# Two heads side by side at lanes 0 to 95, one product for q and k, and token-down tiles spread over three slots

## The chip, the cores and the metric

One Trainium2 chip, of which the program uses one core. The metric is the device time of one execution in microseconds. A kernel's time is the median of its runs.

## The reference

Three layers stand one behind the other, in float32, for 4 batches of 768 tokens.

```python
# attention: q, k, v, alpha are (4, 8, 768, 48)
for t in range(S):
    state = alpha[:, :, t, :, None] * state + einsum('bhd,bhe->bhde', k[:, :, t], v[:, :, t])
    y[:, :, t] = einsum('bhd,bhde->bhe', q[:, :, t], state)
x = y, heads joined: (4, 768, 384)
# mixer
h = maximum(x.T @ w_tok1, 0) @ w_tok2        # over tokens, 768 -> 256 -> 768
u = x + h.T
x2 = u + maximum(u @ w_ch1, 0) @ w_ch2       # over channels, 384 -> 1536 -> 384
# channel mix: xk, xr mix x2 with the token before, weights mu_k, mu_r
out = sigmoid(xr @ w_r) * (maximum(xk @ w_k, 0) ** 2 @ w_v)
```

## The kernel before

**Attention.** A batch is cut into 6 chunks of 128 tokens and 4 pairs of heads: 24 steps. A step works on one pair in one chunk. TensorE transposes q, k and alpha of the pair, so that the head dimension lies along the lanes: head 0 at lanes 0 to 47, head 1 at lanes 64 to 111, with padding (0 for q and k, 1 for alpha) between them. VectorE makes running products of alpha, forwards (`decay`) and backwards (`suffix`), the reciprocal `rlast` of the last decay, and `qd` = q x decay, `kd` = k x suffix (L899 to L911). ScalarE spreads `qd` x `rlast` into a tile of 256 columns, with one head's lanes in the first 128 columns and the other's in the last (`spread_q`, L753); the rest of that tile is zero. TensorE makes the scores of both heads in one product, VectorE masks them into `am` (L928), TensorE computes y from `am`, v and the state (L540, L543) and the chunk's own k-v product from `kdt` (L546). VectorE adds that to the decayed state which GpSimd has made (`state_d`, L420), one instruction a head (L947).

**Precision.** Products in the mixer, and the scores of batches 1 to 3, are made as three products of high and low float32r parts. ScalarE writes the high part (L747, L758, L763, L767), VectorE the low one (L950, L918, L922, L975, L977).

**Mixer.** `token_up` gives two tiles (h1), `token_down` six tiles u (three for each half of the tokens), and 24 channel units follow, each with an up and a down product. The tiles use a ring of two PSUM banks. A token-down tile is six products of 384 columns (L599) and six of 256 columns that add x itself through a shifted identity (L605).

**Order.** Each engine has its own program, written out by hand in 28 slots. Batch 0 has attention alone (a pass of slots before the loop), while the mixer's weights are loaded and split in pieces: ScalarE makes the high part (L729) and GpSimd the low one (L413). Then a loop of three passes interleaves the attention of batch r with the mixer of batch r - 1. In slot s TensorE does the mixer's part, then y of step s - 2, the scores of step s - 1 and the transposes of step s. Slot 0 holds the second token_up tile (the first is made at the end of the pass before), slot 1 nothing of the mixer, slots 2 and 3 three token-down tiles each, and slots 4 to 27 the channel units. ScalarE and VectorE have the second h tile in slot 1, behind the attention of slot 0. The mixer of batch 3 runs alone after the loop, and then the channel mix for all batches.

GpSimd also adds up u (L429) in slots 8 to 13 of a pass. The small `omu` = 1 - mu (L1046) is made on VectorE between batch 0 and the loop.

Of the kernel before, what the change touches and what calls it, by code (L numbers as in the profile page):

```python
# [13 lines left out]
def attention_mixer_channel_mix(nc, q, k, v, alpha, w_tok1, w_tok2, w_ch1, w_ch2,  # L14
# [7 lines left out]
    P = 128  # L22
# [7 lines left out]
    DP = 64  # L30
# [22 lines left out]
    with ctx:  # L53
# [31 lines left out]
        def wr_w(n, kt):  # L85
# [11 lines left out]
        qka = [sb(f"qka{n}", [P, 3, H, DP]) for n in range(2)]  # L97
        vt = [sb(f"vt{n}", [P, NP, 2, W2]) for n in range(2)]
        decay = sb("decay", [P, 4, P])
        suffix = sb("suffix", [P, 2, P])  # L100
# [4 lines left out]
        kd = sb("kd", [P, 2, P])  # L105
# [18 lines left out]
        qka3 = [[buf[:, n, :, :] for n in range(3)] for buf in qka] + [  # L124
            [free_words[half][:, o:o + H * DP].rearrange("p (h d) -> p h d", h=H)
             for half, o in ((0, 0), (0, H * DP), (1, 0))]]
        qbd = free_words[1][:, H * DP:H * DP + 4 * P].rearrange("p (n t) -> p n t", n=2)
        vt3 = vt + [mixed[:, :, :].rearrange("p a t -> p (a t)")[:, 0:NP * 2 * W2]
                    .rearrange("p (a h e) -> p a h e", a=NP, h=2)]
        x2_in = [qka[n][:, :, :, :].rearrange("p a h d -> p (a h d)")[:, 0:KC * (HT + 1)]  # L130
                 .rearrange("p (c t) -> p c t", c=KC) for n in range(2)]
# [10 lines left out]
        def transposed_qka(r, i):  # L142

            b_tr = bank[5] if is_first(r) and i % 2 else bank[0]
            return b_tr[:, 0:P], b_tr[:, P:2 * P], b_tr[:, 2 * P:3 * P]

        def scores_kdT(r, i):

            b_sc = bank[7] if is_first(r) and i % 2 else bank[1]
            return b_sc[:, 0:2 * P], b_sc[:, 2 * P:3 * P]  # L150

        def y_kv(r, i):

            b_y = bank[6] if is_first(r) and i % 2 else bank[2]
            return b_y[:, 0:W2], b_y[:, P:P + W2]
# [18 lines left out]
        qd_ready = sem("qd_ready")  # L174
# [3 lines left out]
        kd_ready = sem("kd_ready")  # L178
# [94 lines left out]
        def _(sp):  # L273
# [95 lines left out]
            sp.wait_ge(consts_v, 14)  # L369
# [13 lines left out]
        def _(pool):  # L383
            def pad(n):

                for a, value in enumerate((0.0, 0.0, 1.0)):
                    nc.gpsimd.memset(qka3[n][a][:, :, D:DP], value).then_inc(consts_g, 1)

            pad(0)
            nc.gpsimd.memset(ident[:, :], 0.0).then_inc(consts_g, 1)  # L390
            pool.wait_ge(consts_g, 4)
            nc.gpsimd.affine_select(out=ident[:, :], in_=ident[:, :], compare_op=ALU.not_equal, fill=1.0,
                                    base=0, pattern=[[-1, P]], channel_multiplier=1).then_inc(consts_g, 1)
            nc.gpsimd.memset(causal[:, :], 1.0).then_inc(consts_g, 1)
            nc.gpsimd.memset(shift_f, 0.0).then_inc(consts_g, 1)
            pad(1)
            pad(2)
            pool.wait_ge(consts_g, 13)

            nc.gpsimd.affine_select(out=causal[:, :].rearrange("p (h t) -> p h t", h=2),  # L400
# [15 lines left out]
            def carry_state(r, i):  # L416
# [3 lines left out]
                nc.gpsimd.tensor_tensor(state_d[:, i % 4, :], state[:, i % NP, :],  # L420
                                        decay[:, i % 4, P - 1:P].to_broadcast([P, W2]), ALU.mult)\
# [57 lines left out]
        def _(pe):  # L479
# [7 lines left out]
            def transposes(r, i):  # L487
                c, p = step(i)
                qb, loads = chunk_buffer(r, c)
                if is_first(r) and i == 0:  # L490
                    pe.wait_ge(consts_g, 5)
                    pe.wait_ge(pair_loaded, 48)
                if is_first(r) and i == 1:
                    pe.wait_ge(consts_g, 15)
                if i % NP == (1 if is_first(r) and i < NP else 0):
                    pe.wait_ge(qka_loaded[qb], 48 * loads)
                if not isinstance(r, int):
                    pe.wait_ge(kd_ready, STEPS * r + i)
                elif i >= 2:
                    pe.wait_ge(kd_ready, i - 1)  # L500
                for n, dst in enumerate(transposed_qka(r, i)):
                    mm = nc.tensor.transpose(  # L502
                        dst, qka3[qb][n][:, 2 * p:2 * p + 2, :].rearrange("p h d -> p (h d)"), ident[:, :])
                mm.then_inc(tr_done, 1)

            def attention_scores(r, i):
                c, _ = step(i)
                pe.wait_ge(kd_ready, STEPS * r + i + 1)
# [6 lines left out]
                if c < NC - 1:  # L515
                    nc.tensor.transpose(kdT, kd[:, i % 2, :], ident[:, :])
                pe.wait_ge(qbd_ready, 2 * (STEPS * r + i + 1))
                if is_first(r):

                    mm = nc.tensor.matmul(scores, kd[:, i % 2, :], qbd[:, i % 2, :], start=True, stop=True)  # L520
                else:
                    pe.wait_ge(split_ready, 3 * (STEPS * (r - 1) + i + 1))
                    for n, (a, b) in enumerate(PASSES):
                        mm = nc.tensor.matmul(scores, ks[a][:, :], qs[b][:, :], start=(n == 0), stop=(n == 2))  # L524
# [598 lines left out]
```

## Time and profile before

| | |
|---|---|
| median of 3 runs | 802.19 us (802.06 to 802.52) |
| the profiled execution | 803.43 us, span 801.8 us |
| mean granted TensorE clock | 0.991 |
| TensorE busy | 776.8 us, 97% |
| VectorE busy | 483.1 us, 60% |
| ScalarE busy | 325.8 us, 41% |
| GpSimd busy | 96.9 us, 12% |
| batch 0's attention | about 5 to 59 us |
| the loop of three passes | about 59 to 468 us |
| mixer of batch 3 | about 468 to 577 us (the channel mix begins inside it) |
| channel mix | to 801.8 us |

A matmul's record begins where its columns start to stream and ends when the last result is out, so records of one engine overlap: the distance between two starts is what a matmul costs. The same holds for VectorE to a smaller degree. A row of the timeline gives the start and the length in us; "x3" means three records in one line, and the square bracket behind it is the engine's idle time before and who ended it.

### The profile page before, as it was taken

What the parts mean: (1) busy time and instruction counts of PE and PEld (TensorE: products, weight loads), DVE (VectorE), ACT (ScalarE), POOL (GpSimd) and SP (SyncE); (2) the same over time, 40 slices, a digit from 0 to 9 for tenths busy, and PEclk for the clock granted to TensorE, in tenths of its full rate; (3) what the DMA queues carried; (4) which work ended last, traced back from release to release, by engine and by line L of the source; (5) the groups of instructions that cost most, each with busy time, mean ns of one, the idle gap of its engine ahead of it and who ended that gap; (6) DMA issues with size and microseconds to landing.
All of it is one profiled execution on the core that took longest, in us unless ns stands there. A gap on an engine that the chain in (4) does not pass through costs nothing.

```text
span 801.8 us, 14717 instructions
## 1 busy us (share of the span) xinstructions
PE 776.8 (97%) x4864; PEld 764.0 (95%) x4864; DVE 483.1 (60%) x1467; ACT 325.8 (41%) x843; POOL 96.9 (12%) x142
## 2 busy tenths in 40 slices
PE   5998999999899999899999999999899999999998
PEld 4887999999899999899999999999899999999998
DVE  6987777872677776367777522243744744753751
ACT  4773433441343333144433313123643733743641
POOL 1665022100002110001210025001000000000000
PEclk9999999999999999999999999999999999999999
DMA  9974222332033232122222002301001101101000
GB/s 189 201 166 78 40 41 40 74 56 44 11 58 49 44 69 40 42 31 40 41 58 75 1 31 76 119 30 42 19 30 50 39 30 50 39 30 57 1 29 29
DMA packets 114895, 43.88 MB, mean 55 GB/s; under 512 B 102160, under 2 KB 112016, under 8 KB 114832
## 3 DMA queue, kind: packets, MB, share of 16 engines
q1 hardware_dynamic: 113680, 38.36, 22.8%
q0 software_dynamic: 1152, 4.72, 1.6%
q8 instruction: 35, 0.57, 0.3%
q14 instruction: 28, 0.23, 0.1%
HBM read 33.63 MB, written 9.44 MB: 54 GB/s over the span
## 4 chain that ended last, share of the span: by engine, by line
PE 85%; DVE 7%; issue 3%; ACT 2%; POOL 1%; DMA 1%; SPq 1%; DVEq 0%; ACTq 0%; POOLq 0%
PE bank L635 19%; PE bank L619 18%; PE bank L701 13%; PE bank L679 11%; PE bank L688 4%; PE bank L540 3%; PE bank L524 3%; PE bank L599 3%; PE bank L502 3%; PE bank L543 2%; PE bank L605 2%; PE bank L546 2%; PE bank L573 2%; DVE decay L899 1%; DMA qka<-in_alpha 1%
## 5 line engine op out<-in xcount | busy, mean ns | idle before, releaser
L758 ACT ACTIVATE qs_hi<-qd,rlast 64x128 fp32r<-64x128 f32 x144 | 57.6, 400 | 141.7 <-DVE qd L909 139.9
L975 DVE SCALAR_TENSOR_TENSOR hid_lo<-bank,hid_hi 128x384 fp32r<-128x384 f32 x96 | 53.1, 553 | 68.3 <-ACT hid_hi L767 68.3
L767 ACT ACTIVATE hid_hi<-bank 128x384 fp32r<-128x384 f32 x96 | 46.6, 485 | 68.9 <-PE bank L619 68.9
L846 ACT ACTIVATE relu_k<-bank 128x384 f32<-128x384 f32 x64 | 31.5, 492 | 102.8 <-PE bank L679 85.1
L619 PE MATMUL bank<-u_hi,wch_hi 128*128 128x384 f32 x288 | 71.1, 355 | 0.0
L918 DVE SCALAR_TENSOR_TENSOR qs_lo<-qd,rlast,qs_hi 64x128 fp32r<-64x128 f32 x144 | 52.3, 364 | 27.9 <-ACT qs_hi L758 25.6
L619 PE MATMUL bank<-u_lo,wch_hi 128*128 128x384 f32 x288 | 66.0, 337 | 0.0
L619 PE MATMUL bank<-u_hi,wch_lo 128*128 128x384 f32 x288 | 65.6, 335 | 0.0
L635 PE MATMUL bank<-hid_lo,wch_hi 128*128 128x384 f32 x288 | 65.5, 334 | 0.0
L635 PE MATMUL bank<-hid_hi,wch_hi 128*128 128x384 f32 x288 | 65.4, 334 | 0.0
L635 PE MATMUL bank<-hid_hi,wch_lo 128*128 128x384 f32 x288 | 65.4, 334 | 0.0
L1090 DVE TENSOR_TENSOR x_half<-bank,x_half 128x384 f32<-128x384 f32 x24 | 13.4, 558 | 77.5 <-PE bank L701 77.5
L502 PE MATMUL bank<-ident,qka 128*128 128x128 f32 x264 | 45.4, 283 | 9.2 <-POOL causal L400 4.1
L747 ACT ACTIVATE x_hi<-bank 128x96 fp32r<-128x96 f32 x96 | 23.9, 249 | 73.1 <-PE bank L546 56.7
L420 POOL TENSOR_TENSOR state_d<-state,decay 128x96 f32<-128x96 f32 x64 | 21.9, 346 | 258.8 <-DVE decay L899 258.8
L1073 DVE TENSOR_TENSOR relu_k<-relu_k 128x384 f32<-128x384 f32 x64 | 35.7, 558 | 27.9 <-ACT relu_k L846 26.4
L540 PE MATMUL bank<-vt,relu_k 128*128 128x96 f32 x352 | 51.4, 268 | 0.6 <-DVE relu_k L928 0.6
L619 PEld LDWEIGHTS bank<-u_lo,wch_hi 128*128 128x128 f32 x288 | 51.7, 188 | 0.0
L619 PEld LDWEIGHTS bank<-u_hi,wch_lo 128*128 128x128 f32 x288 | 51.6, 188 | 0.0
L540 PEld LDWEIGHTS bank<-vt,relu_k 128*128 128x128 f32 x352 | 50.0, 190 | 1.6 <-DVE relu_k L928 1.6
L635 PEld LDWEIGHTS bank<-hid_hi,wch_hi 128*128 128x128 f32 x288 | 51.2, 188 | 0.1
L635 PEld LDWEIGHTS bank<-hid_hi,wch_lo 128*128 128x128 f32 x288 | 51.3, 188 | 0.0
(124 smaller groups left out, 1837.1 us busy)
## 6 DMA issues: line engine op xcount, KB each, us to landing
w_raw<-in_moe_w_ch SPq DMA_DIRECT2D x12, 384.0 KB, 3.7
x_scratch<-x_half POOLq DMA_DIRECT2D x8, 576.0 KB, 3.5
out<-x_half SPq DMA_DIRECT2D x24, 192.0 KB, 1.9
vt<-in_v SPq DMA_DIRECT2D x44, 96.0 KB, 2.5
qka<-in_q SPq DMA_DIRECT2D x21, 192.0 KB, 3.1
qka<-in_k SPq DMA_DIRECT2D x21, 192.0 KB, 3.9
qka<-in_alpha SPq DMA_DIRECT2D x21, 192.0 KB, 4.1
qka<-x_scratch SPq DMA_DIRECT2D x4, 577.5 KB, 3.9
```

The costliest lines, as they stand in the source:

```text
L502: mm = nc.tensor.transpose(dst, qka3[qb][n][:, 2 * p:2 * p + 2, :].rearrange("p h d -> p (h d)"), ident[:, :])
L540: mm = nc.tensor.matmul(y_ps, am[:, i % 2, h * P:(h + 1) * P], vt3[vb][:, p, h, :], start=(h == 0), stop=(h == 1 and c == 0))
L619: mm = nc.tensor.matmul(dst, ch1_w(a, n % KC, jj), u[c][:, n % KC, half * HT:(half + 1) * HT], start=(n == 0), stop=(n == 3 * KC - 1))
L635: mm = nc.tensor.matmul(b_acc[m][:, 0:HT], ch2_w(a, jj, m), hid[c][:, j % HJ, :], start=(jj == 0 and n == 0), stop=(jj == NJ - 1 and n == 2))
L679: mm = nc.tensor.matmul(dst, wk_w(a, n % KC, j), mix_out[0][c][:, n % KC, :], start=(n == 0), stop=(n == 3 * KC - 1))
L688: mm = nc.tensor.matmul(b_acc[m][:, 0:DM], mix_out[1][a][:, n % KC, m * P:(m + 1) * P], wr_w(c, n % KC), start=(n == 0), stop=(n == 3 * KC ...
L701: mm = nc.tensor.matmul(bank[m][:, 0:DM], k2[a][:, n % NF, m * P:(m + 1) * P], wv_w(c, n % NF), start=(n == 0), stop=(n == 3 * NF - 1))
L758: nc.scalar.activation(dst[lanes, h * P:(h + 1) * P], qd[lanes, i % 4, :], ACT.Copy, scale=rlast[lanes, i % 4:i % 4 + 1])\
L767: nc.scalar.activation(dst, b_ring[t % 2][:, 0:HT], func).then_inc(tile_hi, 1)
L918: nc.vector.scalar_tensor_tensor(qs[1][lanes, cols], qd[lanes, i % 4, :], rlast[lanes, i % 4:i % 4 + 1], qs[0][lanes, cols], ALU.mult, ALU ...
L975: ins = nc.vector.scalar_tensor_tensor(dst, src, 0.0, hi, ALU.max, ALU.subtract)
L1073: nc.vector.tensor_tensor(relu_k[:, j % 2, :], relu_k[:, j % 2, :], relu_k[:, j % 2, :], ALU.mult).then_inc(k2_ready, 1)
```

## The change

- The heads of a pair lie unpadded at lanes 0 to 47 and 48 to 95. All per-step tiles use lanes 0 to 95. The padding fills on GpSimd go, and with them TensorE's wait for them.
- Where the code used to pick a head's lanes by their number, it now multiplies by a mask column: `head` (128 x 2) has ones at a head's lanes. A new VectorE instruction makes `rhead` = head x rlast, one column a head. ScalarE's spread and VectorE's low part take it as their scalar over all 96 lanes, and the state update becomes (k-v product x head) + state_d in one instruction.
- `decay` and `suffix` lie side by side, so do q and k in PSUM, and one product of 256 columns makes `qkd`, which holds qd and kd. ScalarE's spread waits for this product.
- `rhead` has to wait for the reciprocal in front of it.
- The token-down tiles are two a slot in slots 1 to 3. In a tile the products with the second h tile come last, behind the residual products. ScalarE and VectorE make the second h tile in slot 0, after that slot's attention.
- Four zero fills before the loop go.

```diff
-        qd = sb("qd", [P, 4, P])
+        rhead = sb("rhead", [P, 4, 2])
+        head = sb("head", [P, 2])
+        qkd = sb("qkd", [P, 4, 2, P])
...
-                if is_first(r) and i == 1:
-                    pe.wait_ge(consts_g, 15)
...
-                    nc.tensor.transpose(kdT, kd[:, i % 2, :], ident[:, :])
+                    nc.tensor.transpose(kdT, kd[0:W2, i % 4, :], ident[0:W2, 0:W2])
...
-                    mm = nc.tensor.matmul(kv_ps, kdt[:, i % 2, :],
+                    mm = nc.tensor.matmul(kv_ps, kdt[:, i % 2, 0:W2],
...
             def token_down(b, half, m):
...
+                for kt in range(KT):
+                    for n, (i, j) in enumerate(PASSES):
...
+                        mm = nc.tensor.matmul(dst, h1[i][:, kt, m * P:(m + 1) * P], tok2_w(j, kt, half),
+                                              start=(kt == 0 and n == 0), stop=(kt == KT - 1 and n == 2))
+                    if kt > 0:
+                        continue
+                    for n in range(TM):
...
 (mixer_part, TensorE)
-                elif s < FIRST_UNIT:
-                    pe.wait_ge(w_lo_ready, TOK2_END)
-                    for m in range(KC):
-                        token_down(b, s - KT, m)
+                elif s < FIRST_UNIT:
+                    if s == 1:
+                        pe.wait_ge(w_lo_ready, TOK2_END)
+                    for n in (2 * s - 2, 2 * s - 1):
+                        token_down(b, *divmod(n, KC))
...
 (spread_q, ScalarE)
-                act.wait_ge(qd_ready, STEPS * r + i + 1)
+                act.wait_ge(qkd_ready, STEPS * r + i + 1)
                 for h in range(2):
-                    lanes = slice(h * DP, (h + 1) * DP)
-                    nc.scalar.activation(dst[lanes, h * P:(h + 1) * P], qd[lanes, i % 4, :], ACT.Copy,
-                                         scale=rlast[lanes, i % 4:i % 4 + 1])\
+                    nc.scalar.activation(dst[0:W2, h * P:(h + 1) * P], qd[0:W2, i % 4, :], ACT.Copy,
+                                         scale=rhead[0:W2, i % 4, h:h + 1])\
...
 (loop pass, ScalarE; VectorE has second_low in the same place)
                     mixer_part(r - 1, s)
                     attention_part(r, s)
+                    if s == 0:
+                        second_high(r - 1)
...
 (scale_qk, VectorE)
-                nc.vector.tensor_tensor(qd[:, i % 4, :], qT, decay[:, i % 4, :], ALU.mult).then_inc(qd_ready, 1)
+                dve.wait_ge(rlast_ready, G + 1)
+                nc.vector.tensor_scalar(rhead[0:W2, i % 4, :], head[0:W2, :], rlast[0:W2, i % 4:i % 4 + 1], None,
+                                        ALU.mult).then_inc(rhead_ready, 1)
                 dve.wait_ge(suffix_ready, G + 1)
-                nc.vector.tensor_tensor(kd[:, i % 2, :], kT, suffix[:, i % 2, :], ALU.mult).then_inc(kd_ready, 1)
+                nc.vector.tensor_tensor(qkd[0:W2, i % 4, :, :],
+                                        transposed_qka(r, i)[:, 0:2 * P].rearrange("p (n t) -> p n t", n=2),
+                                        decays[0:W2, i % 4, :, :], ALU.mult).then_inc(qkd_ready, 1)
...
 (outputs, VectorE)
-                            ins = nc.vector.tensor_tensor(own, kv, state_d[lanes, i % 4, h * D:(h + 1) * D], ALU.add)
+                            ins = nc.vector.scalar_tensor_tensor(own, kv_ps[:, cols], head[0:W2, h:h + 1],
+                                                                 state_d[0:W2, i % 4, cols], ALU.mult, ALU.add)
```

## Rows read from the trace of the kernel before

**Rows 1.** The page's part 1: busy us, share of the span, instructions.

```profile
PE 776.8 (97%) x4864; PEld 764.0 (95%) x4864; DVE 483.1 (60%) x1467; ACT 325.8 (41%) x843; POOL 96.9 (12%) x142
```

**Rows 2.** Windows: us, busy us and instructions of each engine, granted clock, DMA.

```profile
20.00:40.00 20.00, 19.81 (x145) 17.49 (x144) 19.55 (x91) 15.48 (x45) 12.12 (x15) 1.00 1.08 200
...
197.00:223.00 26.00, 23.59 (x149) 22.18 (x147) 15.95 (x53) 9.27 (x26) 0.81 (x1) 0.93 0.19 45
```

**Rows 3.** Timeline, batch 0, VectorE: start us, length us, instruction.

```profile
24.04 0.14 DVE L908 RECIPROCAL rlast<-decay 128x1 f32<-128x1 f32 x1
24.09 0.27 DVE L909 TENSOR_TENSOR qd<-bank,decay 128x128 f32<-128x128 f32 x1
...
24.48 0.41 DVE L947 TENSOR_TENSOR state<-bank,state_d 64x48 f32<-64x48 f32 x2
...
24.92 0.26 DVE L950 TENSOR_TENSOR x_lo<-bank,x_hi 128x96 fp32r<-128x96 f32 x1
...
26.07 0.14 DVE L908 RECIPROCAL rlast<-decay 128x1 f32<-128x1 f32 x1
```

**Rows 4.** Timeline, the second step's transposes.

```profile
7.64 0.87 PE L502 MATMUL bank<-ident,qka 128*128 128x128 f32 x3 [2.66 <-DMA qka<-in_alpha]
```

**Rows 5.** Timeline, head of the second loop pass.

```profile
199.27 1.20 PE L573 MATMUL bank<-x_hi,wtok_lo 128*128 128x384 f32 x6
...
200.78 0.82 ACT L758 ACTIVATE qs_hi<-qd,rlast 64x128 fp32r<-64x128 f32 x2 [5.75 <-DVE qd L909]
...
201.64 0.73 DVE L918 SCALAR_TENSOR_TENSOR qs_lo<-qd,rlast,qs_hi 64x128 fp32r<-64x128 f32 x2 [0.69 <-ACT qs_hi L758]
...
202.60 0.55 DVE L975 SCALAR_TENSOR_TENSOR h_lo<-bank,h_hi 128x384 fp32r<-128x384 f32 x1
...
202.74 0.39 PE L524 MATMUL bank<-qs_hi,ks_hi 128*128 128x256 f32 x1 [1.42 <-DVE ks_lo L922]
...
218.81 0.77 PE L619 MATMUL bank<-u_hi,wch_hi 128*128 128x384 f32 x3
```

**Rows 6.** Timeline, batch 0, ScalarE and GpSimd.

```profile
22.36 0.82 ACT L758 ACTIVATE x_half<-qd,rlast 64x128 f32<-64x128 f32 x2 [0.44 <-DVE qd L909]
...
24.11 0.24 ACT L747 ACTIVATE x_hi<-bank 128x96 fp32r<-128x96 f32 x1
24.13 1.81 POOL L413 TENSOR_TENSOR wtok_lo<-w_raw,wtok_hi 128x768 fp32r<-128x768 f32 x1 [1.65 <-ACT wtok_hi L729]
...
25.91 0.65 POOL L420 TENSOR_TENSOR state_d<-state,decay 128x96 f32<-128x96 f32 x2
```

**Rows 7.** Timeline, between batch 0 and the first loop pass.

```profile
59.15 3.64 POOL L413 TENSOR_TENSOR wch_lo<-w_raw,wch_hi 128x768 fp32r<-128x768 f32 x2 [0.39 <-ACT wch_hi L729]
59.29 1.73 DVE L1046 TENSOR_SCALAR omu<-mu 128x6 f32<-128x6 f32 x1
```

**Rows 8.** Timeline, first token-down tiles of batch 3.

```profile
471.40 0.33 PE L599 MATMUL bank<-wtok_hi,h_hi 128*128 128x384 f32 x1
...
473.71 0.34 PE L599 MATMUL bank<-wtok_hi,h_hi 128*128 128x384 f32 x1
...
475.47 0.44 PE L599 MATMUL bank<-wtok_hi,h_hi 128*128 128x384 f32 x1
```

**Rows 9.** Timeline, slot 4 of the second loop pass.

```profile
220.85 0.69 PE L540 MATMUL bank<-vt,relu_k 128*128 128x96 f32 x4 [0.20 <-DVE relu_k L928]
```

**Rows 10.** Timeline, a steady slot of the first loop pass.

```profile
127.96 0.29 DVE L922 TENSOR_TENSOR ks_lo<-kd,ks_hi 128x128 fp32r<-128x128 f32 x1
...
128.72 0.39 PE L546 MATMUL bank<-vt,relu_k 128*128 128x96 f32 x2
...
128.94 0.27 PE L516 MATMUL bank<-ident,kd 128*128 128x128 f32 x1
...
129.41 0.49 PE L502 MATMUL bank<-ident,qka 128*128 128x128 f32 x3
...
129.66 0.60 PE L619 MATMUL bank<-u_hi,wch_hi 128*128 128x384 f32 x2
```

More of the change, by code:

```diff
@@ L523, in attention_scores @@
                     for n, (a, b) in enumerate(PASSES):
-                        mm = nc.tensor.matmul(scores, ks[a][:, :], qs[b][:, :], start=(n == 0), stop=(n == 2))
+                        mm = nc.tensor.matmul(scores, ks[a][0:W2, :], qs[b][0:W2, :], start=(n == 0), stop=(n == 2))
                 mm.then_inc(scores_done, 1)
@@ L767, in tile_high, with second_high @@
                 nc.scalar.activation(dst, b_ring[t % 2][:, 0:HT], func).then_inc(tile_hi, 1)
+            def second_high(b):
+                tile_high(b, 1, h1[0][:, 1, :], ACT.Relu)
             def mixer_part(b, s):
-                if s < KT:
-                    tile_high(b, s, h1[0][:, s, :], ACT.Relu)
+                if s == 0:
+                    tile_high(b, 0, h1[0][:, 0, :], ACT.Relu)
                 elif s < FIRST_UNIT:
-                    half = s - KT
-                    if half == 0:
+                    if s == 1:
                         act.wait_ge(x2_base, 2 * KC * b + 1)
-                    for m in range(KC):
-                        tile_high(b, KT + KC * half + m, u[0][:, m, half * HT:(half + 1) * HT], ACT.Copy)
+                    for n in (2 * s - 2, 2 * s - 1):
+                        half, m = divmod(n, KC)
+                        tile_high(b, KT + n, u[0][:, m, half * HT:(half + 1) * HT], ACT.Copy)
                 else:
@@ L940, in outputs @@
                     for h in range(2):
-                        lanes = slice(h * DP, (h + 1) * DP)
-                        kv = kv_ps[lanes, h * D:(h + 1) * D]
-                        own = state[lanes, p, h * D:(h + 1) * D]
+                        cols = slice(h * D, (h + 1) * D)
+                        own = state[0:W2, p, cols]
                         if c == 0:
-                            ins = nc.vector.tensor_copy(own, kv)
+                            ins = nc.vector.tensor_scalar(own, kv_ps[:, cols], head[0:W2, h:h + 1], None, ALU.mult)
                         else:
-                            ins = nc.vector.tensor_tensor(own, kv, state_d[lanes, i % 4, h * D:(h + 1) * D], ALU.add)
+                            ins = nc.vector.scalar_tensor_tensor(own, kv_ps[:, cols], head[0:W2, h:h + 1],
+                                                                 state_d[0:W2, i % 4, cols], ALU.mult, ALU.add)
                     ins.then_inc(state_ready, 1)
@@ L1040, in _ @@
                     last_constants()
-            for n in range(2):
-                for h in range(2):
-                    nc.vector.tensor_copy(qs[n][:, h * P:(h + 1) * P], zeros[:, :]).then_inc(consts_v, 1)
-            dve.wait_ge(consts_v, 13)
             dve.wait_ge(mu_loaded, 32)
```

160 lines of the change are left out of this document (81 added, 79 removed).

## The prediction

> **What bounds the kernel now.** I read the page first. TensorE is busy 97% of the span [rows 1]. That number alone says little, since matmuls overlap, so I cut the span into stretches [rows 2] and asked in each which engine never rests. Three kinds of stretch come out.
>
> From 16 to 58 us, the attention of batch 0, VectorE is busy 19.55 of 20 us [rows 2]. The timeline shows it as a chain without a hole: reciprocal follows reciprocal after 2.03 us [rows 3], the same from 16 us to 54.5 us, 19 times. This stretch costs what a VectorE step costs. Before 16 us the loads set the pace: the second transposes wait until 7.64 us for alpha [rows 4].
>
> Inside the three loop passes TensorE has no gaps (steady slots of 4.8 us) except at the head. There the stretch 197 to 223 us shows 23.59 us of work in 26 and a mean granted clock of 0.93 [rows 2]; the head of each pass looks alike. A mean of 0.93 means that twice the missing 0.07, 0.14 x 26 = 3.6 us, ran at 1.2 GHz instead of 2.4, in which half the work is lost, so it costs 1.8 us. It comes directly after TensorE stood waiting.
>
> The last part (mixer of batch 3, feed forward) is TensorE work that the change leaves alone, but for one place.
>
> **The change, part by part.** (a) *The VectorE step in batch 0.* Removed: qd and kd, which together take 24.48 - 24.09 = 0.39 us from start to start [rows 3]. Added: one product of 256 columns. An instruction of 128 columns takes 0.27 us [rows 3], one of 384 takes 0.55 [rows 5]; 256 lie at 0.41, and start to start about 0.08 less as qd shows, so 0.33. Added too: the head-masked scalar rhead, which waits for the reciprocal's own end. The reciprocal takes 0.14 and its successor now starts after 0.05 [rows 3]; with the wait it is 0.14 plus the length of a signal. Between engines that is 0.04 (ScalarE's spread ends at 200.78 + 0.82, qs_lo starts at 201.64 [rows 5]). That makes 0.18, plus rhead's own start to start, 0.05 to 0.12. So recip to state goes from 0.44 to 0.18 + 0.09 + 0.33 = 0.60, that is +0.16. The two state updates and the start of x_lo now take 24.92 - 24.48 = 0.44 [rows 3]; their durations (0.41 for two) leave no overlap, as between different lanes. With all at lane 0 I take the usual overlap: two times 0.18 = 0.36, so -0.08. They now read a per-lane scalar; qs_lo, which does, takes 0.365 against qd's 0.27, so up to +0.1 each. Bounds of the step: 0 and +0.35. I take +0.08.
>
> Two waits follow. ScalarE's x_hi ends at 24.35 and state starts at 24.48 [rows 3, 6]: it has about 0.1 us to spare. ScalarE's spread starts at 22.36 [rows 6], 0.35 us after its reciprocal (one step before the one at 24.04, so at 22.01), and must wait for the whole product, 0.18 + 0.09 + 0.41 + 0.04 = 0.72 after it. So spread, the weight split behind it and x_hi (in the order of ScalarE) slip by 0.37, while state slips by 0.16 + 0.08: a stall of about 0.1 in each step with a weight piece, every second one. And rhead has its only company on GpSimd: state_d behind the long split (25.91 for 0.65 [rows 6]) meets the rhead of the second step; say 0.1 to 0.15 again. Per pair of steps 0.16 + 0.1 + 0.13 = 0.39; some 9 pairs bound by VectorE, so +3.5. Taken off: the four zero fills before the passes, which VectorE doesn't need now, 0.3. **+3.2**, bounds 0 and +8.
>
> A row speaks against rhead. The small omu, 128x6, took 1.73 us and ended as the first of two GpSimd splits ended (59.15 to 60.97) [rows 7]. It is the one other tensor_scalar from SBUF to SBUF, as rhead is. The splits take 1.81 us and start at 24.13, 0.09 after the reciprocal [rows 6]. In the new order the split starts 0.36 later for the spread and rhead 0.18 after its reciprocal, which itself is 0.08 to 0.16 later: rhead is ahead of the split by 0.1 to 0.2 us. I take it that it gets through. The Trainium skill, "SBUF — State Buffer", section Who interferes with whom, says that a tensor_scalar in a two-port mode and a GpSimd instruction lock one shared port pair, and whoever comes first blocks the other for its whole length. The omu row agrees; by that rule the cost hangs on the order of two starts, and is my third rival.
>
> (b) *Loop heads.* Now in slot 0, TensorE ends token_up (a row of six 384-column matmuls lasts 1.20 [rows 5], the last of them 0.34 [rows 8], so one starts every 0.86 / 5 = 0.173; 199.27 + 6 x 0.173 = 200.31), then waits for kd and for ks_lo until 202.74 [rows 5]; only 0.3 us of work lies between. It then runs 3.6 us at half clock. Two slots carry three tiles and slot 1 none; the first channel tile starts at 218.81 [rows 5]. New: at 200.31 tile 0 of token-down can start (its h tile is long done). A tile is 1.76 us [rows 8]; three hi/lo products of 384 columns (0.52) and six residual products (1.76 - 6 x 0.173 = 0.72) go by before it needs the second h tile, at 201.55. ScalarE makes that behind the spread: the spread started at 200.78, now 0.37 later (201.15 to 201.97), ks_hi about 0.2, then 0.49: 202.68. TensorE idles 1.15, does 0.35, and waits for h_lo: VectorE is then at ks_lo, with h_lo behind it (202.60 for 0.55 now [rows 5]) about 0.2 later, until 203.35. It ends the tile at 203.5, the second at 205.3. Slot 1's scores and transposes are 129.66 - 128.72 less kdt's 0.22 = 0.72 [rows 10]; slots 2 and 3 add kdt and four passes of 0.11 for y, 1.38, and two tiles, 4.9 each: 215.8 against 218.81 if the clock stays at 2.4 GHz. Gain 3.0, or 1.2 if it falls as now. The waiting adds up to 1.5 us against 2.1 before; I take it that the clock holds. In pass 1 GpSimd is still splitting weights and rhead and qs_lo wait for it (omu again [rows 7]), and h_lo stands behind them on VectorE and TensorE behind h_lo: gain between 0 and 2, taken 0.9. Sum for three passes **-6.9**, bounds -9 and -2.
>
> Slot 4 has one channel tile only as cover (1.56 us), and TensorE already waits for the mask there (0.20 and a gap before it [rows 9]). The mask comes 0.16 later: **+0.5** for three passes. In steady slots the cover is twice as long: ks_lo ends at 128.25, TensorE comes to the scores behind kd's transpose of 128.94 [rows 10], 0.7 later, and 0.3 of that goes. If that cover were gone, 0.3 x 66 slots = 20 us would be lost; nothing here takes 0.7 away, and it is outside the range like rival three.
>
> (c) *Narrower operands on TensorE.* kdt has 96 weight columns rather than 128: its two passes start at 128.72, the next instruction at 128.94 [rows 10]: 0.22, 0.11 each. The three transposes have 96 weight columns too and still 128 moving: 129.66 - 129.41 = 0.25, 0.083 each. The trace has no narrower weight load. Nothing is the lower bound (moving columns set it), a quarter of both the upper: 0.055 + 0.062 = 0.12 us a step, and 0.01 for kd's transpose. Over 72 steps in gapless passes that is 0 to 9 us. 96 moving columns at 2.4 GHz would be 0.04, so the 0.11 is not their streaming in one pass; I take a third of the bound, 0.04 a step: **-3.0**. The Trainium skill, "TensorE: Matmul & The Clock Gate", section LDWEIGHTS, has the load go with the number of columns, columns / 1.2 ns: 107 ns for 128 and 80 for 96. The 0.11 a pass agrees, the transposes' 0.083 doesn't. By the page, as an estimate, kdt and transposes would give 5 x 0.027 = 0.13 a step, all of my upper bound, and the sum would be 6 us lower.
>
> (d) *Mixer of batch 3.* Its first token-down tile takes 473.71 - 471.40 = 2.31 us against 1.76 for the next [rows 8]; it waits for the second h tile. The residual products now stand in that wait: **-0.55**.
>
> (e) *Nothing:* the fills of the pads and the wait for them (the DMA of [rows 4] comes later); masks, 96 instead of 128 lanes on ScalarE, VectorE and GpSimd, since an instruction's time goes by its columns (two copies of 64 lanes x 48 columns take 0.41 [rows 3], one of 128 x 128 takes 0.27); DMAs, which move the same rows. The state updates in the passes become unlocked too, off the path.
>
> **Sum.** +3.2 - 6.9 + 0.5 - 3.0 - 0.55 = -6.8 us. The profiled execution had a span of 801.8 and a time of 803.43; the median of the runs is 802.19, 1.24 lower. From the median: 802.19 - 6.8, rounded to 795.
>
> **The rivals.** *Two: the gain at the heads is eaten.* TensorE still waits 1.5 us per head; if that lets the clock fall, passes 2 and 3 give 1.2 each and pass 1 nothing: 2.4. With the batch 0 step at +0.2 (+5) and no gain from narrow weights: 802.19 + 5 - 2.4 + 0.5 - 0.55 = 804.7; with (a) as taken and 1.5 from (c), 801.4. For it: the clock falls in all three heads now. Against: the wait is shorter and broken by work. I put it at 802.
>
> *Three, slower: rhead falls behind the weight split.* Place: the batch 0 steps with a piece. If rhead's start is later than the split's start, VectorE stands for what is left of 1.81 us. Some 10 pieces there x 1.7 = 17: 795 + 17 = 812. It decides at 0.1 to 0.2 us: one more signal delay of that size on VectorE does it. For it: omu. Against: the order that I worked out.
>
> *Four: narrow operands pay in full.* (c) at -8.5 and (a) at +1.5: 802.19 + 1.5 - 6.9 + 0.5 - 8.5 - 0.55 = 788. For it: both TensorE blocks are slower than their moving columns. The rule of the Trainium skill named in (c) leads here.
>
> **How the numbers follow.** Forecast 0.48, rival two 0.21, three 0.15, four 0.16. The range reaches from rival four's far side, 787, to 803 above rival two, and leaves out three and slivers. The forecast's own range is 790 to 799. 0.2% is 1.6 us, about what a measurement can tell. Faster by more: forecast and four, and half of two, less a little: 0.73. Within: 0.10. Slower: rival three and the end of two: 0.17.
>
> **What would show it.** Batch 0: reciprocals 2.2 us apart instead of 2.03, rhead about 0.18 after the reciprocal with a length near 0.1 (1.8 if rival three). Heads: one TensorE wait of about 1.2 us inside the first token-down tile and one of 0.3; granted clock 1.0 in all 26 us (0.93 if rival two); from first transposes to first channel tile 19 us instead of 22. Steady slots of 4.75 instead of 4.79 us; kdt passes below 0.11. Wrong would be: state updates with a mask much dearer than copies, rhead held up, a wait for ks_lo in the steady slots.

## The result, and the profile after

The kernel is 1.3% slower: 812.6 us (median of 4 runs, 811.34 to 812.82) against 802.2 (802.06 to 802.52), ratio 1.0126, 95% interval 1.0108 to 1.0143. The forecast was 795.0 with a range of 787 to 803; what came is its third rival, priced at 812 and given 0.15. The profiled execution has a span of 810.8 us against 801.8, so the spans differ by 9.0.

To see where they lie I took, on TensorE, the first transposes of each pass and the first token_up product of batch 3's mixer. Before, pass 1 begins at 59.32 us and batch 3's mixer at 468.28; after, at 78.25 and 477.94. So batch 0 grew by 18.93 us, the three passes shrank by 9.27 (408.96 to 399.69), and the rest shrank by 0.66. The heads of passes 2 and 3 are as forecast, that of pass 1 gains more; batch 0 lost almost twice what all the rest gained.

Windows of the kernel after: two in batch 0, and the head of pass 2, which begins at 212.27 here, for the 197 to 223 of [rows 2] (us, busy us and instructions of PE, PEld, DVE, ACT, POOL, granted clock, DMA):

```profile
20.00:40.00 20.00, 14.85 (x95) 12.49 (x95) 19.79 (x61) 9.04 (x30) 8.96 (x11) 0.91 0.67 142
40.00:64.00 24.00, 21.38 (x122) 18.45 (x123) 23.51 (x76) 12.12 (x39) 9.55 (x12) 0.79 0.59 147
212.00:238.00 26.00, 24.34 (x162) 23.13 (x163) 18.20 (x62) 9.05 (x30) 1.15 (x2) 1.00 0.19 48
```

VectorE is as full as before (19.79 of 20), but with 61 instructions where [rows 2] had 91: they have become long, or one has. The head of pass 2 has the granted clock at 1.00 instead of 0.93.

Timeline of VectorE in batch 0 after, for [rows 3] (start us, length us, instruction):

```profile
23.05 0.13 DVE L909 RECIPROCAL rlast<-decays 96x1 f32<-96x1 f32 x1
23.22 0.22 DVE L914 TENSOR_SCALAR rhead<-head,rlast 96x2 f32<-96x2 f32 x1
23.35 0.41 DVE L917 TENSOR_TENSOR qkd<-bank,decays 96x256 f32<-96x256 f32 x1
23.69 0.43 DVE L955 SCALAR_TENSOR_TENSOR state<-bank,head,state_d 96x48 f32<-96x48 f32 x2
24.04 0.24 DVE L959 TENSOR_TENSOR x_lo<-bank,x_hi 128x96 fp32r<-128x96 f32 x1
...
25.18 0.13 DVE L909 RECIPROCAL rlast<-decays 96x1 f32<-96x1 f32 x1
25.35 1.79 DVE L914 TENSOR_SCALAR rhead<-head,rlast 96x2 f32<-96x2 f32 x1
27.05 0.41 DVE L917 TENSOR_TENSOR qkd<-bank,decays 96x256 f32<-96x256 f32 x1
...
28.87 0.13 DVE L909 RECIPROCAL rlast<-decays 96x1 f32<-96x1 f32 x1
```

The same rhead of two elements a lane takes 0.22 us in one step and 1.79 in the next. A free step is 25.18 - 23.05 = 2.13 us long, the held one 28.87 - 25.18 = 3.69. Of the last 20 of batch 0's 24 steps ten are held (1.78 to 1.80 us, one 1.42), of the first four none. ScalarE and GpSimd in the same stretch, for [rows 6]:

```profile
23.80 0.69 ACT L754 ACTIVATE x_half<-qkd,rhead 96x128 f32<-96x128 f32 x2 [0.88 <-DVE qkd L917]
24.40 0.83 ACT L726 ACTIVATE wtok_hi<-w_raw 128x768 fp32r<-128x768 f32 x1
```

```profile
25.31 1.80 POOL L411 TENSOR_TENSOR wtok_lo<-w_raw,wtok_hi 128x768 fp32r<-128x768 f32 x1 [2.07 <-ACT wtok_hi L726]
```

GpSimd's split starts at 25.31, rhead at 25.35, and rhead ends as the split ends. In nine of the ten held steps the split is ahead by 0.03 or 0.04 us; in the one of 1.42 it is ahead by 0.41, and there too rhead ends as the split ends. In the passes a GpSimd instruction of 1.01 us (the residual preparation) holds rhead in six slots of each:

```profile
121.99 0.35 POOL L418 TENSOR_TENSOR state_d<-state,decays 96x96 f32<-96x96 f32 x1 [4.39 <-DVE decays L900]
...
122.23 1.10 DVE L914 TENSOR_SCALAR rhead<-head,rlast 96x2 f32<-96x2 f32 x1
...
122.30 1.01 POOL L427 TENSOR_TENSOR x_half<-u_hi,u_lo 128x384 f32<-128x384 f32 x1
```

Here rhead starts 0.07 us ahead of the long instruction and is held all the same: it starts 0.24 inside state_d's product, and GpSimd goes on to the long one without a gap. In the slots where state_d's product (0.34) stands alone, rhead takes 0.22 or 0.23. So a start ahead of the long instruction need not be enough when GpSimd is already at work. The slots with the residual preparation last 4.86 us where their neighbours last 4.75.

Head of pass 2 after, for [rows 5] (TensorE, with the idle time ahead of an instruction and who ended it in brackets):

```profile
212.27 0.53 PE L498 MATMUL bank<-ident,qka 128*96 128x128 f32 x3 [0.60 <-issue]
218.05 0.44 PE L595 MATMUL bank<-wtok_hi,h_hi 128*128 128x384 f32 x1 [0.88 <-ACT h_hi L762]
...
231.36 0.78 PE L616 MATMUL bank<-u_hi,wch_hi 128*128 128x384 f32 x3
```

From the first transposes to the first channel tile it is 231.36 - 212.27 = 19.09 us; before it was 218.81 - 196.80 = 22.01, the transposes there being these:

```profile
196.80 0.54 PE L502 MATMUL bank<-ident,qka 128*128 128x128 f32 x3 [0.73 <-issue]
```

In the steady slots kdt's pair goes by faster, for [rows 10]:

```profile
110.67 0.33 PE L542 MATMUL bank<-vt,relu_k 128*96 128x96 f32 x2
110.84 0.25 PE L512 MATMUL bank<-ident,qkd 96*128 96x96 f32 x1
...
111.31 0.49 PE L498 MATMUL bank<-ident,qka 128*96 128x128 f32 x3
```

0.17 us for the pair against 0.22. Batch 3, for [rows 8]: the first token-down tile lasts 482.81 - 481.06 = 1.75 us instead of 2.31.

```profile
481.06 0.33 PE L595 MATMUL bank<-wtok_hi,h_hi 128*128 128x384 f32 x1
...
482.81 0.33 PE L595 MATMUL bank<-wtok_hi,h_hi 128*128 128x384 f32 x1
```

### The profile page after: what moved, and what is told of

Same layout as the page of the kernel before. It is cut to its first block, busy times and chain, and to the rows that moved or that the text cites. A ratio compares the mean times of both kernels' runs of the same rounds, so it can differ in the third digit from the quotient of the medians.

```text
span 810.8 us, 14704 instructions
## 1 busy us (share of the span) xinstructions
PE 780.6 (96%) x4864; PEld 764.8 (94%) x4864; DVE 509.8 (63%) x1462; ACT 303.5 (37%) x843; POOL 96.1 (12%) x136
## 4 chain that ended last, share of the span: by engine, by line
PE 87%; DVE 6%; issue 3%; ACT 2%; SPq 1%; DMA 1%; DVEq 0%; ACTq 0%
PE bank L632 19%; PE bank L616 18%; PE bank L698 13%; PE bank L676 11%; PE bank L536 4%; PE bank L685 4%; PE bank L520 4%; PE bank L498 3%; PE bank L595 3%; PE bank L539 2%; PE bank L602 2%; PE bank L569 2%; PE bank L542 1%; PE bank L516 1%; DVE decays L900 1%
## 5 line engine op out<-in xcount | busy, mean ns | idle before, releaser
L754 ACT ACTIVATE qs_hi<-qkd,rhead 96x128 fp32r<-96x128 f32 x144 | 50.1, 395 | 172.6 <-DVE qkd L917 172.6
L927 DVE SCALAR_TENSOR_TENSOR qs_lo<-qkd,rhead,qs_hi 96x128 fp32r<-96x128 f32 x144 | 45.9, 358 | 30.5 <-ACT qs_hi L754 30.5
L914 DVE TENSOR_SCALAR rhead<-head,rlast 96x2 f32<-96x2 f32 x96 | 53.2, 555 | 3.5
L536 PEld LDWEIGHTS bank<-vt,relu_k 128*128 128x128 f32 x352 | 51.9, 196 | 2.1 <-DVE relu_k L937 2.0
L418 POOL TENSOR_TENSOR state_d<-state,decays 96x96 f32<-96x96 f32 x64 | 22.0, 344 | 257.8 <-DVE decays L900 257.8
L498 PE MATMUL bank<-ident,qka 128*96 128x128 f32 x264 | 45.6, 283 | 7.1 <-DMA qka<-in_alpha 6.0
L632 PEld LDWEIGHTS bank<-hid_lo,wch_hi 128*128 128x128 f32 x288 | 51.3, 188 | 0.0
```

Of the source, the lines that this page charges most:

```text
L498: mm = nc.tensor.transpose(transposed_qka(r, i)[:, n * P:(n + 1) * P], qka3[qb][n][:, 2 * p:2 * p + 2, :].rearrange("p h d -> p (h d)"), i ...
L536: mm = nc.tensor.matmul(y_ps, am[:, i % 2, h * P:(h + 1) * P], vt3[vb][:, p, h, :], start=(h == 0), stop=(h == 1 and c == 0))
L632: mm = nc.tensor.matmul(b_acc[m][:, 0:HT], ch2_w(a, jj, m), hid[c][:, j % HJ, :], start=(jj == 0 and n == 0), stop=(jj == NJ - 1 and n == 2))
L754: nc.scalar.activation(dst[0:W2, h * P:(h + 1) * P], qd[0:W2, i % 4, :], ACT.Copy, scale=rhead[0:W2, i % 4, h:h + 1])\
L914: nc.vector.tensor_scalar(rhead[0:W2, i % 4, :], head[0:W2, :], rlast[0:W2, i % 4:i % 4 + 1], None, ALU.mult).then_inc(rhead_ready, 1)
L927: nc.vector.scalar_tensor_tensor(qs[1][0:W2, cols], qd[0:W2, i % 4, :], rhead[0:W2, i % 4, h:h + 1], qs[0][0:W2, cols], ALU.mult, ALU.subt ...
```

## The experiments

Three theories were open for batch 0. A: rhead waits for GpSimd, and the order of two starts decides. B: VectorE's added work and its dependent wait fill batch 0, held or not. C: TensorE's lower granted clock in batch 0 (0.79 to 0.91) lengthens its steps. For the part that gained, the question was whether the tiles did it or the rest of the change. Diffs are against the changed kernel unless said otherwise.

**rhead read from two tiles.** The mask is 0 or 1, so the result is the same number.

```diff
-                nc.vector.tensor_scalar(rhead[0:W2, i % 4, :], head[0:W2, :], rlast[0:W2, i % 4:i % 4 + 1], None,
-                                        ALU.mult).then_inc(rhead_ready, 1)
+                nc.vector.scalar_tensor_tensor(rhead[0:W2, i % 4, :], head[0:W2, :], rlast[0:W2, i % 4:i % 4 + 1],
+                                               head[0:W2, :], ALU.mult, ALU.mult).then_inc(rhead_ready, 1)
```

> rhead is made by an instruction of VectorE in the same place and with the same waits, but it reads two tiles (mask column times 1/d times the mask again, which is 0 or 1), where the changed kernel's reads one tile and a column of scalars. Theory A, the ten long rheads: in the changed kernel rhead takes 0.22 us alone and 1.79 us where GpSimd's split of a weight has started before it, and if only the one-tile form waits for GpSimd, rhead is short in all 20 steps here. Ten times 1.57 us come back, and some 2 us more in the passes, where 18 rheads beside the residual preparation take 1.10 us: 794 to 796 us, transposes of pass 1 begin near 62. Theory B, VectorE's own work (one more instruction a step and the dependent wait ahead of it) fills batch 0: that is unchanged here, 812. Theory C, the lower granted clock of TensorE in batch 0 (0.79 to 0.91) makes the steps long: the clock and the time stay, 812. If the two-tile form is held up as well, the time stays at 812 with rheads of 1.8 us, and the run says nothing against A.

Measured: 813.03 us, ratio to before 1.0122 (1.0105 to 1.0139), the same as the changed kernel. This form is held as well, with the split at 25.33:

```profile
25.37 1.78 DVE L914 SCALAR_TENSOR_TENSOR rhead<-head,rlast 96x2 f32<-96x2 f32 x1
```

So my guess that only the one-tile form waits was wrong, and the run decides nothing between A and B. It does speak against C: the granted clock in 20 to 40 us was 0.74 here against 0.91 in the changed kernel, and the steps are as long (2.12 free and 3.70 held, one of 4.06). The Trainium skill, "SBUF — State Buffer", section Who interferes with whom, lists an instruction of VectorE with two SBUF inputs among those that contend with GpSimd; this row agrees (1.78 us), and had I read that line closely the run would have been spared.

**rhead made by ScalarE.**

```diff
 (scale_qk, VectorE)
-                if is_first(r) and i == 0:
-                    dve.wait_ge(consts_g, 7)
-                dve.wait_ge(rlast_ready, G + 1)
-                nc.vector.tensor_scalar(rhead[0:W2, i % 4, :], head[0:W2, :], rlast[0:W2, i % 4:i % 4 + 1], None,
-                                        ALU.mult).then_inc(rhead_ready, 1)
...
 (spread_q, ScalarE)
+                act.wait_ge(rlast_ready, STEPS * r + i + 1)
+                nc.scalar.activation(rhead[0:W2, i % 4, :], head[0:W2, :], ACT.Copy,
+                                     scale=rlast[0:W2, i % 4:i % 4 + 1]).then_inc(rhead_ready, 1)
+                act.wait_ge(rhead_ready, STEPS * r + i + 1)
                 act.wait_ge(qkd_ready, STEPS * r + i + 1)
```

> rhead is made by ScalarE, ahead of its wait for the two products, and VectorE does not make it at all. Theory A: no instruction of VectorE meets GpSimd's split any more, and VectorE is rid of the instruction and of its wait (0.13 + 0.22 us a step): a step of batch 0 of 1.9 to 2.0 us instead of 2.13 alone and 3.69 beside a split, 788 to 793 us. Theory B says 1.9 to 2.0 us a step as well, so this run alone does not tell A from B; it does together with the two-tile one. Theory C: 812. Against all: ScalarE now has one more instruction ahead of the spread, and if it is the engine that sets the step in the passes, the 60 steps grow by up to 0.2 us, 800 us or above.

Measured: 788.5 us, ratio 0.9822 (0.9805 to 0.9838). Steps of batch 0 are 1.94 us in the mean, and pass 1 begins at 57.23. The instruction takes 0.29 us on ScalarE, inside a split too (27.36, in the split of 27.26 to 29.08):

```profile
27.26 1.82 POOL L411 TENSOR_TENSOR wtok_lo<-w_raw,wtok_hi 128x768 fp32r<-128x768 f32 x1 [1.46 <-ACT wtok_hi L726]
...
27.36 0.29 ACT L754 ACTIVATE rhead<-head,rlast 96x2 f32<-96x2 f32 x1
```

As A and B said alike. The rival about ScalarE in the passes falls: the slots are 4.75 us, with the residual preparation too.

**The split 0.2 us later.** One small copy to a spare tile stands ahead of each rounding of a weight piece in batch 0; rhead is untouched.

```diff
 (batch 0, ScalarE)
                 attention_part(0, s)
                 for n in pieces_in(s):
+                    nc.scalar.activation(spare[:, n % 32, :], head[:, :], ACT.Copy)
                     split_hi(n)
```

> Nothing is changed in rhead; ScalarE has one small copy to a spare tile (0.2 us) ahead of each rounding of a weight piece in batch 0, so that GpSimd's split of the piece starts some 0.2 us later. It leaves the computation as it is. Theory A with the order of the two starts deciding (in the changed kernel the split starts 0.03 to 0.04 us ahead of rhead in the ten long cases): rhead is ahead now and short, 795 to 799 us. Theory A without the order (rhead waits whenever a split runs at any time of it): rhead overlaps the split's start and takes most of 1.8 us again, 812. Theories B and C: 812, or a little more for the added copy.

Measured: 796.63 us, ratio 0.993 (0.9914 to 0.9947), 16.0 us below the changed kernel, though ScalarE has an instruction more for each piece. VectorE and GpSimd:

```profile
24.28 0.22 DVE L916 TENSOR_SCALAR rhead<-head,rlast 96x2 f32<-96x2 f32 x1
...
26.41 0.41 DVE L916 TENSOR_SCALAR rhead<-head,rlast 96x2 f32<-96x2 f32 x1
```

```profile
24.34 1.85 POOL L412 TENSOR_TENSOR wtok_lo<-w_raw,wtok_hi 128x768 fp32r<-128x768 f32 x1 [1.98 <-ACT wtok_hi L727]
26.14 0.65 POOL L419 TENSOR_TENSOR state_d<-state,decays 96x96 f32<-96x96 f32 x2
```

rhead now starts 0.06 us ahead of the split and takes 0.22; starting 0.04 behind it, it took 1.79. That is the order of the starts, and theory B, whose work is all still here, falls: the steps are 2.13 us, and 2.32 in the six where state_d's two products, one behind the other (0.65), hold the next rhead for 0.2. One rhead (at 44.17) also starts inside a product of state_d, 0.06 us ahead of a split that follows without a gap, as in the passes, and yet takes 0.22; no run shows what sets it apart. The 18 holds in the passes are left (1.09 us, slots of 4.86).

**The tiles alone, on the kernel before.** Only token_down's new order, two tiles a slot in slots 1 to 3, and the second h tile behind slot 0's attention; the heads stay padded and q and k apart.

```diff
-                if s < KT:
-                    if s == 0:
-                        token_up(b, 1)
+                if s == 0:
+                    token_up(b, 1)
                 elif s < FIRST_UNIT:
-                    pe.wait_ge(w_lo_ready, TOK2_END)
-                    for m in range(KC):
-                        token_down(b, s - KT, m)
+                    if s == 1:
+                        pe.wait_ge(w_lo_ready, TOK2_END)
+                    for n in (2 * s - 2, 2 * s - 1):
+                        token_down(b, *divmod(n, KC))
```

> The kernel before with the rearranged token-down tiles alone: heads padded to lanes 0 and 64 as they were, no merged product, no rhead. My reading of the two traces: the loop heads give 2.9 to 4.0 us each, less 0.5 for slot 4, 8.0 to 8.7 us in the three passes, and 0.6 in batch 3: 793 to 794.5 us, with batch 0 as before (transposes of pass 1 near 59.3). Rival: the shorter heads of the changed kernel came from the rest of the change (the queue of VectorE is shorter), and the tiles alone give under 3 us: 799 to 802.

Measured: 793.17 us, ratio 0.9878 (0.9861 to 0.9894): 9.1 us off, so the rival falls. In the profiled executions (793.9 against 801.8) the passes last 401.8 us against 408.96 and batch 0 is as before (59.17). So the tiles alone carry 7.2 of the 9.27 us by which the changed kernel's passes shrank, and the 0.6 in batch 3.

**rhead as two instructions of one column.**

```diff
+                for h in range(2):
+                    ins = nc.vector.tensor_scalar(rhead[0:W2, i % 4, h:h + 1], head[0:W2, h:h + 1],
+                                                  rlast[0:W2, i % 4:i % 4 + 1], None, ALU.mult)
+                ins.then_inc(rhead_ready, 1)
```

> rhead is made in the same place by two instructions of one column each (96x1) where the changed kernel has one of two columns (96x2). The two-input form was held up as long as the one-input form (1.78 us), so what the instruction reads beside the mask is not what counts; every other instruction of VectorE in batch 0 reads a bank, or has a single element a lane: the reciprocal (96x1, from SBUF) takes 0.13 us even inside GpSimd's work. Theory D, one element a lane is not held up: two short instructions in all 20 steps, the 10 waits of 1.57 us gone, 0.1 us a step more for the second instruction, 795 to 798 us. Theory E, whatever reads and writes SBUF alone waits for GpSimd, and the reciprocals were only ahead of the split: 812, perhaps with the wait at the reciprocal in other steps.

Measured: 796.8 us, ratio 0.9935 (0.9913 to 0.9958). The pair takes 0.33 us though it starts 0.04 behind the split, as the held ones of the changed kernel do:

```profile
24.53 0.33 DVE L915 TENSOR_SCALAR rhead<-head,rlast 96x1 f32<-96x1 f32 x2
```

```profile
24.49 1.81 POOL L411 TENSOR_TENSOR wtok_lo<-w_raw,wtok_hi 128x768 fp32r<-128x768 f32 x1 [2.05 <-ACT wtok_hi L726]
```

Theory D holds, E falls: engine, form, place and data are the same, and what differs is one element a lane instead of two. The changed kernel has a row that agrees: a reciprocal (96x1, SBUF alone) that started 0.24 us inside a split (at 58.35) took 0.13. Each step pays 0.11 us for the second instruction (2.24), and in the passes the slots with the residual preparation take 4.75 as their neighbours do. Pass 1 begins at 65.09, 4.5 us later than in the next kernel. The steps are 2.5 of it: the last product of q and k starts at 58.34 against 55.86. The other 2.0 lie behind it, where the granted clock was 0.50 (1.2 GHz) in 60 to 65 us; why it fell there and not in the next kernel was not tried.

**The mask read from a bank.** It is copied once into two free columns of the transposes' banks.

```diff
+                head_ps = (bank[5] if is_first(r) and i % 2 else bank[0])[:, 3 * P:3 * P + 2]
+                if is_first(r) and i < 2:
+                    nc.vector.tensor_copy(head_ps, head[:, :]).then_inc(head_copied, 1)
+                    dve.wait_ge(head_copied, i + 1)
-                nc.vector.tensor_scalar(rhead[0:W2, i % 4, :], head[0:W2, :], rlast[0:W2, i % 4:i % 4 + 1], None,
+                nc.vector.tensor_scalar(rhead[0:W2, i % 4, :], head_ps[0:W2, :], rlast[0:W2, i % 4:i % 4 + 1], None,
                                         ALU.mult).then_inc(rhead_ready, 1)
```

> rhead is the same one instruction of two columns in the same place, but it reads the mask from two free columns of the bank that its step's transposes lie in (copied there once) and not from SBUF. Theory F, an instruction of VectorE that reads a bank is never held up by GpSimd, as the products, the mask copies and the state steps of batch 0 show: rhead 0.22 us in all steps, 794 to 797 us. Theory G, the size or form of the instruction alone is what holds it: ten rheads of 1.8 us again, 812.

Measured: 792.31 us, ratio 0.9888 (0.986 to 0.9916), 20.3 us below the changed kernel and 1.7 below the range expected for F. Again 0.04 us behind a split, and free:

```profile
28.06 1.82 POOL L412 TENSOR_TENSOR wtok_lo<-w_raw,wtok_hi 128x768 fp32r<-128x768 f32 x1 [1.82 <-ACT wtok_hi L727]
```

```profile
28.10 0.21 DVE L919 TENSOR_SCALAR rhead<-bank,rlast 96x2 f32<-96x2 f32 x1
```

Pass 1 begins at 60.59, so without the hold batch 0 costs 1.27 us more than before: steps of 2.12 and none held. F holds. That leaves 18.93 - 1.27 = 17.7 us, in two parts. Up to the last product of q and k (71.50 in the changed kernel, 55.86 here) it is 15.6, of which the ten holds are 15.3 (nine of 1.57 and the short one of 1.2). The other 2.0 come behind it, up to pass 1 (6.75 us against 4.73, for the same work): there TensorE, which had waited 2.38 us for the last spread, ran at half clock. The changed kernel first, then this one:

```profile
72.00:78.25 6.25, 5.47 (x21) 5.07 (x21) 1.72 (x7) 3.47 (x8) 2.48 (x2) 0.50 0.40 128
```

```profile
57.00:60.59 3.59, 3.37 (x20) 2.85 (x21) 1.30 (x5) 2.35 (x6) 2.48 (x3) 1.00 0.41 110
```

The windows of the steps settle theory C:

```profile
20.00:40.00 20.00, 18.71 (x140) 16.11 (x138) 19.68 (x86) 12.91 (x43) 11.69 (x15) 1.00 0.89 192
40.00:64.00 24.00, 21.72 (x148) 19.26 (x149) 19.59 (x82) 15.21 (x45) 15.71 (x12) 1.00 0.60 160
```

The clock is at 1.00 here, where TensorE need not stand through the holds. In the changed kernel it was at 0.91 and 0.79, but VectorE, with hardly a gap in 20 to 40 us, set the steps, and a free step has the same 2.12 or 2.13 us at either clock. So in the steps the clock followed and cost nothing; what it cost is the 2.0 us behind them.

**kdt with 128 stationary columns again.**

```diff
-                    mm = nc.tensor.matmul(kv_ps, kdt[:, i % 2, 0:W2],
+                    mm = nc.tensor.matmul(kv_wide(r, i), kdt[:, i % 2, :],
```

> The changed kernel with the two kdt products of a step back at 128 stationary columns (96 now); nothing else. My reading: a pair takes 0.17 us in the changed kernel and took 0.22 in the one before, TensorE is full in the passes, so 0.05 us in each of 60 steps are lost again: 3 us, 815 to 816. Rival: the gain of the steady slots (4.80 to 4.75 us) came from elsewhere (the state steps and the spread of VectorE and ScalarE being shorter): no change, 812.

Measured: 815.15 us, ratio 1.016 (1.0134 to 1.0185), 2.6 us above the changed kernel. The runs of the two spread over 811.3 to 812.8 and 813.0 to 815.5; the profile says it more surely:

```profile
111.44 0.39 PE L546 MATMUL bank<-vt,relu_k 128*128 128x96 f32 x2
111.67 0.25 PE L516 MATMUL bank<-ident,qkd 96*128 96x96 f32 x1
```

0.23 us for the pair against 0.17, and free slots of 4.81 against 4.75. Slots with a held rhead hardly grow (4.87): there VectorE sets the slot, and a faster TensorE buys nothing. (A zero fill before batch 0 grows with this edit too.)

**ScalarE's rhead, and the second h tile ahead of the spread.** Diff against the kernel of 788.5 us; VectorE makes the tile's low half ahead of split_low in the same way.

```diff
 (loop pass, ScalarE)
                     mixer_part(r - 1, s)
-                    attention_part(r, s)
                     if s == 0:
                         second_high(r - 1)
+                    attention_part(r, s)
```

> rhead on ScalarE, as in the kernel of 788.5 us, and in slot 0 ScalarE makes the second h tile ahead of the spread of its step, VectorE its low half ahead of the low halves of q and k. In the changed kernel TensorE waits 0.88 and 0.3 us in the first token-down tile of each pass for that h tile. If the tile's lateness sets the head: 2 to 3.5 us less, 785 to 786.5. Rival: the spread is later by the tile's 0.6 us, and the scores of the next slot wait as long: 788 to 789, the wait only moved.

Measured: 783.65 us, ratio 0.9769 (0.9747 to 0.9791): 4.9 us below that kernel, 18.5 below the one before, the fastest here, and a little below the 785 to 786.5 that I expected. Pass 1 (from its first transposes to those of pass 2) goes from 135.15 to 131.47 us, pass 2 from 132.18 to 130.59. The large share is pass 1's. With the tile late, TensorE waited there, and its clock was at 0.70 in 64 to 69 us:

```profile
64.87 0.45 PE L595 MATMUL bank<-wtok_hi,h_lo 128*128 128x384 f32 x1 [2.45 <-DVE h_lo L985]
```

With the tile early that wait is gone, the clock is 1.00 in 57 to 66 us, and the longest wait there is this one, for the scores, which the tiles now cover:

```profile
64.69 0.38 PE L520 MATMUL bank<-qs_hi,ks_hi 96*128 96x256 f32 x1 [0.19 <-DVE ks_lo L932]
```

## Why the prediction was wrong, step by step

**The step that failed** stands in (a): "rhead is ahead of the split by 0.1 to 0.2 us. I take it that it gets through". It is behind by 0.04. Its own start was right (0.17 us after the reciprocal, forecast 0.18), and so was the spread's (0.75 after it, forecast 0.72). What I left out is that the spread itself gets shorter, which (e) had put at nothing: its two instructions of 64 lanes started at lanes 0 and 64 and took 0.82 us; with 96 lanes each, both starting at lane 0, they overlap to 0.69, and the rounding behind them starts 0.60 after the spread instead of 0.85. Before, on ScalarE, beside the spread at 22.36 of [rows 6]:

```profile
23.21 0.84 ACT L729 ACTIVATE wtok_hi<-w_raw 128x768 fp32r<-128x768 f32 x1
```

From the spread's start to the split's it was 24.13 - 22.36 = 1.77 and is 25.31 - 23.80 = 1.51. These 0.26 us turn a lead of 0.1 to 0.2 into the measured lag. I had used just this overlap for VectorE's two state steps and not for ScalarE. The readings show the shorter time; that it is the lanes that make it was not tried by itself.

Behind it stands a second fault, of judgement. The margin was a tenth of a microsecond, made of several estimated terms, each uncertain by about as much, and the price of losing it was 17 us. I gave it 0.15 and left it outside the range. A term with that ratio of price to margin is a toss, and the range had to reach it. The price was right in size: 17 forecast for ten holds, 15.6 measured up to the last of them, and 2.0 more at half clock behind them, which the forecast had not. That rival three's 812 came within 1 us is partly luck: its terms were too high by 1.4 us for the holds, 1.9 for batch 0 without them, 0.5 for slot 4 and 2.4 for the head of pass 1, and it lacked the 2.0 of half clock and 2.0 of holds in the passes, which I had not thought of. The residual preparation costs there 6 slots x 0.11 x 3 = 2.0 us, shown by the slots of 4.75 instead of 4.86 in each kernel whose rhead isn't held.

**(a) without the hold:** +3.2 forecast, +1.3 measured (the mask from a bank). The step grew by 0.09 us (0.08 forecast), 2.12 or 2.13 for 2.03, and the stalls I had added for x_hi and state_d are not there. Where rhead reads SBUF and is ahead of the split (the later split), state_d's is there, 0.2 us in six steps for the 0.1 to 0.15 forecast, and batch 0 costs +2.7 (pass 1 begins at 62.00). The masked state steps cost hardly more than the plain ones (0.43 for two against 0.41).

**(b) heads:** -6.9 + 0.5 forecast. The tiles alone shortened the three passes by 7.2. In pass 2, 2.92 was measured for 3.0, by the steps named: a wait inside the first tile (0.88 for 1.15), a second of about 0.3, and a clock that holds at 1.00. Rival two falls. The +0.5 for slot 4 did not come: from its first channel tile to the next slot's it was 222.94 - 218.81 = 4.13 us and is 235.47 - 231.36 = 4.11.

In pass 1, 3.3 was measured (from 23.24 to 19.9) against 0.9 forecast, and 1.9 of it go with the late start of the pass. In the four kernels whose pass 1 begins by 62.0 us with the h tile in its place behind the spread (ScalarE's rhead, the later split, the tiles alone, the mask from a bank) the same stretch lasts 21.8 to 22.0 us, a gain of 1.2 to 1.5; in the four that come there at 65.1 us or later (the changed kernel, the two tiles, the single columns, the wide kdt) it lasts 19.7 to 20.3. TensorE's wait for h_lo is a little shorter in the changed kernel (2.06 us, against 2.46 with the mask from a bank), and its granted clock stays at 1.00 (84 to 90 us), against 0.72 (66 to 72 us) there. So part of what the late start of pass 1 cost came back at its head; why the clock held was not tried.

**(c) narrower operands:** -3.0 forecast; kdt is worth 2.6 in the runs and 0.055 us a free slot, so the size is right, but its make-up is not: I had spread it over kdt and transposes. All of it is kdt, 0.085 a pass instead of 0.11. The three transposes with 96 weight columns still take 0.25 (93.00 to 93.25). The Trainium skill's rule in "TensorE: Matmul & The Clock Gate", section LDWEIGHTS, fits kdt (107 to 80 ns by the page, 110 to 85 here) and not the transposes, so rival four falls.

**(d) batch 3:** -0.55 forecast, -0.56 measured. **(e)** held but for the spread on ScalarE, above.

**The sum.** The passes gave 9.27 against 9.4 forecast, though with 2.0 lost in them that I hadn't seen and 2.4 won in pass 1. The case that the forecast of 795.0 describes, rhead from SBUF and ahead of the split, is the kernel with the later split: 796.6. With no hold anywhere (the mask from a bank) it is 792.3, but 1.6 us of its gain in the profiled execution lie behind batch 3's first tile, in work that the change leaves alone; the granted clock was 1.00 in its channel mix (560 to 700 us) and 0.99 before (568 to 708 us).

What stays open: by what means the bank's and the single column's rhead escape (the runs show only that they do), why rhead is held when it starts just ahead of a long instruction but inside a short one (in the 18 slots of the passes, though not at 44.17 of the later split), why the spread's two instructions overlap more, and why the clock fell behind batch 0 in some kernels and held at the head of pass 1 in others.

## What to carry to other kernels

An instruction of VectorE that touches SBUF alone can cost, even with two elements a lane, as much as the longest instruction on GpSimd. When you add one, list what runs on GpSimd in that stretch, the short instruction ahead of the long one too, and do not rest the cost on an order of two starts; read one operand from a bank, work on one element a lane, or give it to ScalarE. When a change moves an instruction's lanes or width, redo the times of every engine in the race, those that get faster too. And a bet with a margin of 0.1 us and a price of 17 belongs inside the range.

## What the runs showed of the hardware that I had not expected

- 0.1 us of order decides the hold: rhead 0.06 us ahead of the split, with GpSimd idle, took 0.22 us, 0.04 behind it 1.79. With GpSimd at work the order is no guarantee: 0.24 us inside state_d's product and 0.07 ahead of the 1.01 us behind it, rhead took 1.10.
- What was held and what was not, in the same place 0.04 us behind a split: 96x2 from SBUF by tensor_scalar (1.79) and by scalar_tensor_tensor (1.78) were; two of 96x1 (0.33 together) and 96x2 with its tile input in a bank (0.21) were not. On ScalarE, 0.29 inside a split.
- Two ScalarE instructions of 128 columns took 0.82 us when they started at lanes 0 and 64 (64 lanes each), and 0.69 when both started at lane 0 (96 lanes each).
- 96 stationary columns shorten kdt's pass from 0.11 to 0.085 us and a transposes' pass not at all (0.083).
- A free slot shows a saving on TensorE (0.055 us) and a slot in which VectorE is held does not, in the same pass.
